# Attention steps beside the first dense expert: two pairs of heads per place instead of one

## What is computed

```python
scores = q @ k.T / 8;  mask: 0 <= i - j < 64;  attn = softmax(scores)
x   = (attn @ v)                                     # 1152 x 512
out = sum_e p[:, e] * (relu(x @ w1[e]) @ w2[e])      # 4 dense experts, 512 -> 1024 -> 512
# then 8 routed experts: y = relu(x @ u1[e]) @ u2[e] on each row's own expert, gated, added to x
```

## Time and profile before

| what | value |
|---|---|
| median of 3 runs | 632.85 us (632.48 to 632.9) |
| the profiled execution's own time | 632.4 us |
| its span, first to last instruction | 630.8 us |
| PE busy | 617.9 us (98%) |
| DVE busy | 291.9 us (46%) |
| ACT busy | 245.6 us (39%) |
| POOL busy | 76.0 us (12%) |
| granted TensorE clock, mean | 0.997 |

### The profile page before, as it was taken

How to read it: one execution, slowest core, us unless ns; L and a number is a source line. 1 busy time by engine, 2 the same in 40 slices (tenths; PEclk the granted TensorE clock), 3 DMA queues, 4 the chain that set the end, 5 groups by cost and what they waited for, 6 DMA issues and landing times.

```text
span 630.8 us, 9697 instructions
## 1 busy us (share of the span) xinstructions
PE 617.9 (98%) x3433; PEld 549.9 (87%) x3434; DVE 291.9 (46%) x760; ACT 245.6 (39%) x520; POOL 76.0 (12%) x121
## 2 busy tenths in 40 slices
PE   8999999999999999999999999999999999999995
PEld 7889999898989898989899998989888888888884
DVE  5575566524512124512124333344567744771681
ACT  5765545421402013301113221232345764863771
POOL 6660000000000000000000001010011321231221
PEclk9999999999999999999999999999999999999998
DMA  8744234008999994210002331033567857693541
GB/s 280 216 132 118 61 92 158 12 1 231 235 263 220 257 260 157 85 48 0 0 0 66 94 108 67 11 111 118 172 219 282 266 153 245 206 363 73 169 154 22
DMA packets 51314, 90.27 MB, mean 143 GB/s; under 512 B 13128, under 2 KB 17736, under 8 KB 51280
## 3 DMA queue, kind: packets, MB, share of 16 engines
q1 hardware_dynamic: 47088, 82.15, 43.9%
q0 software_dynamic: 3520, 7.53, 4.8%
q10 hardware_dynamic: 672, 0.15, 0.1%
HBM read 64.15 MB, written 27.08 MB: 145 GB/s over the span
## 4 chain that ended last, share of the span: by engine, by line
PE 95%; DVE 2%; ACT 1%; issue 1%; DMA 1%; POOL 0%; SPq 0%; DVEq 0%; POOLq 0%; ACTq 0%
PE ps_h L1173 31%; PE ps_y L1173 31%; PE ps_y L1262 11%; PE ps_h L1262 10%; PE ps_s L1071 2%; PE ps_o L1116 2%; PE ps_s L1277 2%; PE ps_s L1150 1%; PE ps_t L1086 1%; PE ps_h L1197 1%; PE ps_t L1251 1%; DMA qz<-q 1%; PE ps_t L1138 1%; ACT prob L627 0%; PE ps_h L1059 0%
## 5 line engine op out<-in xcount | busy, mean ns | idle before, releaser
L700 ACT ACTIVATE ht_hi<-ps_h 128x384 fp32r<-128x384 f32 (+1 forms) x104 | 48.6, 467 | 235.9 <-PE ps_h L1173 229.0
L1173 PE MATMUL ps_h<-xt_hi,w_hi_a 128*128 128x384 f32 (+1 forms) x400 | 130.9, 327 | 0.0
L1173 PE MATMUL ps_h<-xt_hi,w_lo_a 128*128 128x384 f32 (+1 forms) x400 | 129.4, 324 | 0.0
L1173 PE MATMUL ps_h<-xt_lo,w_hi_a 128*128 128x384 f32 (+1 forms) x400 | 129.3, 323 | 0.0
L1173 PE MATMUL ps_y<-w_hi_a,ht_hi 128*128 128x512 f32 x288 | 115.5, 401 | 0.0
L1173 PE MATMUL ps_y<-w_hi_a,ht_lo 128*128 128x512 f32 x288 | 112.7, 391 | 0.0
L1173 PE MATMUL ps_y<-w_lo_a,ht_hi 128*128 128x512 f32 x288 | 112.4, 390 | 0.0
L931 DVE SCALAR_TENSOR_TENSOR ht_lo<-ps_h,ht_hi 128x384 fp32r<-128x384 f32 (+1 forms) x104 | 54.7, 526 | 119.1 <-ACT ht_hi L700 118.8
L1173 PEld LDWEIGHTS ps_h<-xt_hi,w_hi_a 128*128 128x128 f32 x400 | 75.4, 188 | 0.5 <-DVE ht_lo L931 0.2
L1173 PEld LDWEIGHTS ps_h<-xt_lo,w_hi_a 128*128 128x128 f32 x400 | 75.4, 188 | 0.4
L1173 PEld LDWEIGHTS ps_h<-xt_hi,w_lo_a 128*128 128x128 f32 x400 | 75.3, 188 | 0.0
(11 more groups left out here) (176 smaller groups left out, 830.7 us busy)
## 6 DMA issues: line engine op xcount, KB each, us to landing
raw<-u SPq DMA_DIRECT2D x36, 512.0 KB, 4.7
x_sorted<-xg SPq DMA_DIRECT2D x4, 4112.0 KB, 43.6
raw<-w SPq DMA_DIRECT2D x32, 512.0 KB, 4.6
x<-u SPq DMA_DIRECT2D x24, 512.0 KB, 6.0
vt<-v SPq DMA_DIRECT2D x17, 256.0 KB, 2.9
xg<-x_sorted POOLq DMA_DIRECT2D x13, 257.0 KB, 6.0
kt<-k SPq DMA_DIRECT2D x8, 384.0 KB, 4.1
x_sorted<-xg SPq DMA_DIRECT2D x1, 2313.0 KB, 44.5
```

Of the source, the lines that this page charges most:

```text
L700: a.activation(ht_hi[:, pos, 0:P * tiles], ps_h[:, pos % 2, 0:P * tiles], ACT.Relu).then_inc(h_hi_done, 1)
L1173: ins = mm(dst, hi_lo[l], rhs_hi_lo[r], start=(first and n == 0), stop=(last and n == 2))
```

## The change

The places beside the first expert no longer carry steps but *groups*: group g is the steps 2g and 2g + 1. At a place PE does four score products of group g, then four transposes of group g - 1 into the whole of `ps_t`, then four output products of group g - 2. ACT copies `ps_t` with one 128x512 copy, and it stands between the exponentials of step 2g and of step 2g + 1. DVE's part is split over two positions: masks of both steps and `normalise(2g)` at the place, `normalise(2g + 1)` and the two `xt_lo` at the position after (`group_end`). There are 16 places (6, 4, 6) where there were 31 (11, 8, 12): chunk 0 at positions 0, 3, 7, 11, 15, 19, chunk 1 at 0, 5, 11, 17, chunk 2 at 0, 3, 7, 11, 15, 19. The second layer's high weights in chunk 0 move to positions 2, 4, 5, 6. The prologue is as it was.

```diff
-            for i, pos in enumerate((3, 4, 5, 7)):
+            for i, pos in enumerate((2, 4, 5, 6)):
...
+    def groups_for(tiles):
+        return PAIRS * tiles // 2 + 2
+    GROUPS = PAIRS * NT // 2
+    FIRST_GROUP = PAIRS * FIRST_CHUNKS[0][1] // 2
...
-            for n, step in enumerate(steps):
-                at.setdefault(n * room // len(steps), []).append(step)
+            for n, g in enumerate(range(begin, end)):
+                pos = n * room // (end - begin)
+                at.setdefault(pos, []).append(("group", g))
+                at.setdefault(pos + 1, []).append(("group_end", g))
...
+            # ACT
+            def group(g):
+                if g < GROUPS:
+                    scores(2 * g)
+                if FIRST_GROUP <= g - 1 < GROUPS:
+                    act.wait_ge(pt_ready, 2 * g)
+                    act.wait_ge(pv_done, 2 * g - 2)
+                    copy(prob_t[:].rearrange("p r s n -> p (r s n)"), ps_t[:]).then_inc(pt_copied, 2)
+                if g < GROUPS:
+                    scores(2 * g + 1)
+                if FIRST_GROUP <= g - 2:
+                    act.wait_ge(pv_done, 2 * g - 2)
+                    for j in range(2):
+                        dst, src = outputs(xt_hi, 2 * g - 3, j)
+                        copy(dst, src).then_inc(xt_hi_done, 1)
...
+            # DVE
+            def group(g):
+                if g < GROUPS:
+                    mask_scores(2 * g)
+                    mask_scores(2 * g + 1)
+                    normalise(2 * g)
+            def group_end(g):
+                if g < GROUPS:
+                    normalise(2 * g + 1)
+                if FIRST_GROUP <= g - 2:
+                    for j in range(2):
+                        dve.wait_ge(xt_hi_done, 2 * g - 3 + j)
+                        dst, src = outputs(xt_lo, 2 * g - 3, j)
+                        minus_hi(dst, src, outputs(xt_hi, 2 * g - 3, j)[0]).then_inc(xt_split, 1)
...
+            # PE
+            def group(g):
+                if g < GROUPS:
+                    scores(2 * g)
+                    scores(2 * g + 1)
+                if FIRST_GROUP <= g - 1 < GROUPS:
+                    pe.wait_ge(probs_normal, 4 * g)
+                    pe.wait_ge(pt_copied, 2 * g - 2)
+                    for i in range(2):
+                        for half in range(HALVES):
+                            n0 = P * (2 * i + half)
+                            last = turn(ps_t[:, n0:n0 + P], prob[:, (4 * g - 4 + 2 * i + half) % BUFFERS, :], ident[:])
+                        last.then_inc(pt_ready, 1)
+                if FIRST_GROUP <= g - 2:
+                    t = (2 * g - 4) // PAIRS
+                    pe.wait_ge(pt_copied, 2 * g - 2)
+                    pe.wait_ge(values_landed[t % 2], 16 * 2 * (t // 2 + 1))
+                    pe.wait_ge(xt_split, 2 * g - 4)
+                    for r in (2 * g - 4, 2 * g - 3):
+                        a = r % PAIRS
+                        for half in range(HALVES):
+                            n0 = P * (2 * (r % 2) + half)
+                            last = mm(ps_o[:, n0:n0 + P], vt[:, t % 2, half, P * a:P * a + P], prob_t[:, r % 2, half, :],
+                                      start=True, stop=True)
+                        last.then_inc(pv_done, 1)
```

More of the change, by code:

```diff
@@ L93, in beside_first @@
         if c < len(FIRST_CHUNKS) - 1:
-            begin, end = (steps_for(sum(FIRST_CHUNKS[i])) for i in (c, c + 1))
+            begin, end = (groups_for(sum(FIRST_CHUNKS[i])) for i in (c, c + 1))
             room = FC + FIRST_CHUNKS[c][1] * FC - 1
-            steps = [("attention", p) for p in range(begin, end)]
             if c == 0:
-                steps = [("scores", p) for p in range(begin - LAG - 1, begin)] + steps
-            for n, step in enumerate(steps):
-                at.setdefault(n * room // len(steps), []).append(step)
+                begin = FIRST_GROUP
+            for n, g in enumerate(range(begin, end)):
+                pos = n * room // (end - begin)
+                at.setdefault(pos, []).append(("group", g))
+                at.setdefault(pos + 1, []).append(("group_end", g))
         return at
@@ L628, in scores @@
                                  accum_out=sums[:, u % BUFFERS:u % BUFFERS + 1]).then_inc(probs_ready, 1)
-                if p == PROLOGUE - 1:
-                    copy_probs(EARLY)
             def copy_probs(r):
@@ L683, in beside @@
                         attention(*what[1:])
-                    elif what[0] == "scores":
-                        scores(*what[1:])
+                    elif what[0] == "group":
+                        group(*what[1:])
                     elif what[0] == "first_weights":
@@ L912, in beside @@
                         attention(*what[1:])
-                    elif what[0] == "scores":
-                        scores(*what[1:])
+                    elif what[0] == "group":
+                        group(*what[1:])
+                    elif what[0] == "group_end":
+                        group_end(*what[1:])
                     elif what[0] == "weights":
@@ L1074, in scores @@
                 last.then_inc(scores_ready, 1)
-                if p == PROLOGUE - 1:
-                    turn_probs(EARLY)
             def turn_probs(r):
@@ L1162, in beside @@
                 for what in at.get(pos, []):
[L1163 to L1166, removed]
+                    if what[0] == "group":
+                        group(*what[1:])
                     elif what[0] == "route":
```

## The result

The changed kernel takes 634.62 us (median of 8 runs, 634.29 to 635.4), the kernel before 632.66 us in the same session: a ratio of 1.0032, 95% interval 1.0023 to 1.0042. It is slower by 2.0 us; the forecast was 634.4, 1.55 us above the kernel before. The profiled execution shown here is the slowest of the eight; its own time is 635.4 us.

A forecast was written before the change was run, and what follows sets the result against it. PE, busy 98% of the span, bounds the kernel. Chunk 0's -0.1 and +1.65 from chunks 1 and 2 (2.73 new waits against 1.08 going) give +1.55 us on 632.85, so 634.4, range 632.7 to 635.8.

The forecast's parts named there:

- the base: The median of the kernel before, 632.85 us, to which the forecast added its +1.55 us.
- A place costs 1.11 and changing kinds nothing: On PE: a full place costs 1.11 us, a group place 2.22; changing between attention and dense products costs nothing visible.
- Old waits that go: PE's waits in the kernel before, 2.9 us: 1.86 in chunk 0 and 1.08 in chunks 1 and 2 were to go.
- the four of 0.37: Four places whose outputs wait for DVE to empty the one bank ps_o; each 0.37 us was to go.
- the 0.24: Hidden stage, third block after the full place at 62.51: an old wait of 0.24 us with its restart, to go.
- The one in chunk 0: Chunk 0's worst old place, losing 1.12 us on xt_lo; position 11's group was to come 0.85 late after the change.
- one more place: One more place of the kernel before, counted among the old waits as losing some 0.1 us.
- New waits: Hidden stage, chunks 1 and 2: block pos + 3 loses 0.41, block pos + 4 0.75 with restart; 2.73 us in sum.
- Chunk 0: Block 3 waits 0.9 behind a normalising slowed by POOL, position 11's group 0.85: 1.75 against 1.86 going, net -0.1 us.
- The sentence that the moved weight pieces hide: Chunk 0: weight pieces moved a position earlier cost nothing, ready by 33 us while PE wants them after 38.
- Outside the chunks: Beyond chunks 0 to 2 the forecast had no term; loads of keys and values were to cost nothing.

The follow-up runs named there:

- e6: The changed kernel with four slots in prob_t instead of two and the two xt_lo a position later; 632.01 us, ratio 0.9986 to the kernel before.
- e1: The changed kernel with four slots in prob_t instead of two, so ACT's copy no longer waits for its own place's outputs; 632.83 us, ratio 1.0002.
- e5: The changed kernel with the two xt_lo a position later, behind the evacuation of block pos + 2; 633.56 us, ratio 1.0016.
- e2: The changed kernel with groups at positions 5, 9, 13, 17, 21 in chunks 1 and 2, five in each; 632.57 us, ratio 0.9996.
- e3: The changed kernel with the second layer's four high weight pieces back at positions 3, 4, 5, 7; 635.04 us, ratio 1.004.
- e4: The changed kernel with the normalising of step 8 (chunk 0's first group) behind block 1's evacuation instead of ahead of it; 634.74 us, ratio 1.0031.
- the padded kernel: The kernel before with already met semaphore waits added ahead of each second-layer product group of the first expert; 632.43 us, ratio 0.9992.
- e8: The kernel before with ACT making xt_hi ahead of the prob_t copy instead of behind it, from chunk 0 on; 631.67 us, ratio 0.9981.

## Why the prediction was right

*The size.* 634.4 forecast, 634.62 measured; in the three chunks +1.55 forecast, +1.51 measured. That it is so close is partly luck. Terms of the sum were off by a few tenths and cancel: chunk 0 came out 0.2 lower than said, the new waits of the hidden stage 0.13 lower, and a wait of 0.35 at group 18 was not in the sum. And the 0.4 to 0.5 us outside the chunks, on which I did not count, is in part hidden by the base: I added to 632.85, and the kernel before took 632.66 beside the result.

*A place costs 1.11 and changing kinds nothing.* Right: 4.99 us from place to place, and e6's chunk 1 without waits.

*Old waits that go.* Right for the four of 0.37 and the 0.24. The one in chunk 0 became 0.8, as allowed for (0.85). The "one more place" of 0.1 did not go but grew: it is the place in chunk 2 that has no scores left ahead of its transposes. I walked only places with scores. Group 18 has none, so its outputs come 0.9 earlier and wait for the bank after all, 0.35 with the restart:

```profile
118.35 0.60 PE L1165 MATMUL ps_t<-ident,prob 128*128 128x128 f32 x4
119.07 1.13 PE L1177 MATMUL ps_o<-prob_t,vt 128*128 128x128 f32 x8
```

*New waits.* Right in place and cause, block by block (3 and 4 in chunk 1; 3, 6 and 7 in chunk 2). In size 0.46 and 0.60 were measured for 0.41 and 0.75: ACT's chain was 0.05 longer than walked (`ht_lo` ends 5.40 into the place, not 5.35), DVE's normalising 0.1 shorter, 0.79 to the next start and not 0.89, because the end of one instruction overlaps the next. 2.60 for 2.73 in the sum; e1 removes the three at block pos + 3, e5 the two at block pos + 4, and e2 all five by other places.

*Chunk 0.* The sum was near (waits 0.3 less than before, I said 0.1 less), and block 3 waited 0.67 for 0.9, behind a normalising that ran beside POOL's products, as in the earlier trace rows (two multiplications of 1.22 us together, where the next two, with POOL idle, take 0.48):

```profile
27.41 1.22 DVE L859 TENSOR_SCALAR prob<-prob,sums 128x128 f32<-128x128 f32 x2
28.55 0.41 DVE L967 SCALAR_TENSOR_TENSOR ht_lo<-ps_h,ht_hi 128x256 fp32r<-128x256 f32 x1
```

The sentence that the moved weight pieces hide held, but its reasons were too few, and e3's expectation, which called the move neutral, was wrong. I asked whether POOL would have the low weights in time, and looked on ACT only at the first piece; at the old position the piece stands ahead of a group's whole work on ACT and delays a block by 0.7. It did no harm to the sum because the changed kernel has the new positions. And e4 shows that the wait at block 3 is no term of its own: taken away, it returns at block 6.

*Outside the chunks* I expected nothing, and 0.4 to 0.5 us of the difference between the medians is there, with its cause open.

## What to carry to other kernels

Work that hides beside a saturated engine is paid for by position: ask of every instruction put into a side engine's queue which evacuation stands behind it, and how many blocks ahead PE is by then. A copy that must wait for the products of its own place (here because two slots are filled at once) holds everything behind it; a second pair of slots (1.7 us) and moving two instructions behind the next evacuation (1.2) turned a loss of 1.5 us in the chunks into a gain of 1.4. Before restructuring to remove a wait, try the order within the queue that ends it: two lines exchanged in the kernel before gave 0.8 us in the trace's chunks. Its medians differ by 1.4 (ratio 0.9981), but 0.6 of that need not be its own: the padded kernel, with chunks as before, lies 0.6 under the same median. The groups in their best form (e6) win more in the chunks, 1.4, and no more in the medians (ratio 0.9986, with intervals that overlap).

## What the runs showed of the hardware

The start of the program differs from trace to trace. In that of the kernel before the first score products, at 5.81, take 0.76 to the next row, and from 6.79 a pair of them takes 0.45; in that of the changed kernel they take 0.99:

```profile
6.79 0.61 PE L1071 MATMUL ps_s<-kt,qz 128*128 128x128 f32 x4
7.24 0.39 PE L1059 MATMUL ps_h<-xr 128*128 128x128 f32 x2
```

```profile
6.14 1.20 PE L1107 MATMUL ps_s<-kt,qz 128*128 128x128 f32 x4 [0.62 <-DMA qz<-q]
7.13 0.63 PE L1095 MATMUL ps_h<-xr 128*128 128x128 f32 x2
```

One product of the next row (x2) takes 0.22 in the first (7.24 to 7.46) and 0.42 in the second (7.13 to 7.55): about twice the distance is TensorE at 1.2 instead of 2.4 GHz. In the changed kernel's trace it stays so until 10.4 us, in the other until 6.3; before that PE had waited 0.62 and 0.30 us for the first queries. The first dense block starts at 23.17 there instead of 22.18. In five of the 13 traces, all with changed code, the clock is up only at 9.7 to 10.9 us, and they start the block at 23.13 to 23.44. In the traces of e5 and e6 the clock is up at 6 and the block still starts at 23.30 and 23.16, but there PE waits for a load of keys, 0.73 and 0.61 us. In e6:

```profile
11.65 0.71 PE L1112 MATMUL ps_s<-kt,qz 128*128 128x128 f32 x4 [0.61 <-DMA kt<-k]
```

The six traces with neither start it at 22.18 to 22.51. So a late start goes with one of the two. What makes the clock rise late isn't shown: e1 waited 1.3 us for its queries, longer than any of the five, and had the clock up at 4.2.

In the traces the length of the routed stage goes with where PE's instructions stand. It is 147.77 to 147.84 us in the three traces with the old layout of PE's instructions (the two of the kernel before, and e8, which changes only ACT's) and 148.12 to 148.43 in the ten others, the padded kernel among them. Most of it is lost in the second slot: at its start in the changed kernel (0.43) and in the padded one (0.21), in the changed kernel's second trace in small parts, and in e2 and e3 4 us later in the same slot (0.27 and 0.31). The second slot is the first that PE takes from a loop; whether that is the reason isn't shown.
